# Spreading the four store transfers of a transposed group over four attention units, and one unit's sum moved ahead of another's shift

## The chip, the cores and the metric

The kernel runs on one core of one Trainium2 chip, alone. The metric is the device time of one execution in microseconds (us); the kernel before takes 838.05 us, the median of three runs (835.47, 838.05 and 839.6). The profile is of one further execution, which took 836.59 us; 834.8 us of that is the span from its first to its last instruction.

## The reference, cut to what matters

Three stages follow each other. Attention: 4 batches, 8 heads, 768 positions, head size 64, in chunks of 32 queries that see a window of 64 keys (8 memory keys, 16 on the left, the chunk itself, 8 on the right).

```python
scores = scale * np.matmul(q_c, k_full.transpose(0, 1, 3, 2))
scores = scores - np.max(scores, axis=-1, keepdims=True)
a = np.exp(scores)
a = a / (np.sum(a, axis=-1, keepdims=True) + 1e-09)
out[:, :, c_start:c_end] = np.matmul(a, v_full)
```

Its output, as x with 3072 tokens of 512 features, goes through two dense blocks:

```python
h = x @ w_in                                   # 512 -> 1024
solu = h * softmax(h)
ln = (solu - mean) / np.sqrt(var + 1e-06) * g_ln
x = ln @ w_out                                 # 1024 -> 512
g = np.maximum(0.01 * (x @ w_in2), x @ w_in2)  # 512 -> 2048
out = g @ w_out2                               # 2048 -> 512
```

## The kernel before, in words

The attention is cut into 32 units of work: eight blocks of 384 tokens times four pairs of heads. The first dense product (step `hidden`), the softmax and the normalization run over 24 tiles of 128 tokens, three per block. Every fp32 product of the dense blocks is made of three products of split operands (high and low parts).

All engines take their work from one list of steps, written out by hand: `START` for the first block, `BLOCK_STEPS` for each further block, `TAIL` for the end (lines 106 to 202). `schedule()` puts them together, and each engine walks the same list and does the steps that it has in its own table (`run`, line 443). So the order within an engine is fixed, and engines meet only at semaphores.

One attention unit a goes like this. SyncE (SP) issues `load_q(a)`, `load_k(a)`, `load_v(a)`: 192, 384 and 384 KB. `load_q` goes to one of two buffers `q_raw`; the other two go to one of four slots of `attn_buf`. GpSimd (POOL) copies q into the slot with zeros between heads (`place_q`, line 1386, two copies at line 1399). TensorE (PE) makes the scores (line 695); VectorE (DVE) takes the maximum away (`shift`, lines 1139 to 1146); ScalarE (ACT) does `expo` (line 861); DVE sums and inverts (`rsum`, lines 1155 to 1157); POOL multiplies (`probs`, line 1407); PE transposes (`probs_t`, line 707); ACT spreads the result over a diagonal layout (`spread`); PE multiplies by the values (`values`, line 721); ACT and DVE take the high and low part of the result (`x_hi`, `x_lo`).

In `BLOCK_STEPS` POOL's work stands in this order for block t, counted in units from 4t: place 8, probs 4, place 9, probs 5, probs 6, place 10, place 11, probs 7, with the small steps of the normalization (`stats`, `stats_a`) between. POOL is in order, so a `place_q` that waits for its q holds up the `probs` behind it. SP is in order too: `load_v(a)` waits until `values(a-4)` has read the slot, `load_q(a)` until `place_q(a-2)` has read the buffer, `load_k(a)` until `scores(a-4)` is done.

After normalization DVE transposes each tile in squares of 32 (`tr`, line 1181) into `lnT`, which has two buffers of four tiles (a group, 2 MB). Six groups are written to DRAM: `store_ln(g)` (line 477) waits for the group's last transpose and issues four transfers, each of 32 partitions, 512 KB, with 512 bytes of contiguous DRAM per piece. `tr` of the first tile of group g+2 waits until all four transfers of group g have landed. In `schedule()` the whole `store_ln(g)` is put behind the first `scores` step that is more than 24 steps after the group's last `tr`; the last two groups are put directly behind their last `tr` in `TAIL`. `load_ln` later reads the groups back for the second dense product.

At the very beginning PE multiplies zeros (`keep_warm`, line 838) while the first loads arrive: 10, 6 and 12 matmuls, which the profile counts as 20, 12 and 24.

Of the kernel before, what the change touches and what calls it, by code (L numbers as in the profile page):

```python
# [22 lines left out]
P = 128  # L23
# [11 lines left out]
HALVES = TOKENS // HALF  # L35
NT = BLOCKS * TILES
GROUP = HALF // P
SQUARE = 32
# [63 lines left out]
def down_count(b, p, j=PAIRS2 - 1):  # L102
# [2 lines left out]

START = (
        ("keep_warm", 10), ("place_q", 0),
        ("scores", 0), ("keep_warm", 6), ("load_q", 4), ("load_k", 4), ("place_q", 1), ("shift", 0),
        ("scores", 1), ("keep_warm", 12), ("load_q", 5), ("load_k", 5), ("expo", 0), ("place_q", 2), ("shift", 1), ("rsum", 0), ("expo", 1), ("rsum", 1), ("probs", 0), ("w1_hi", 0), ("probs", 1),
        ("probs_t", 0), ("spread", 0), ("w1_lo", 0),  # L110
        ("scores", 2), ("load_q", 6), ("load_k", 6), ("place_q", 3),
        ("values", 0), ("load_v", 4), ("shift", 2),
# [94 lines left out]
def schedule():  # L207


    s = []  # L210

    def add(*steps):
        s.extend(steps)


    def x2_steps(h, k):
        add(("x2", h, k))
        if k == 3 and h >= 1:
            for m in range(KM):
                add(("stage_x2", h - 1, m))  # L220
            add(("store_x2", h - 1))
        if k % 2 == 1 and h + 2 < HALVES:
            add(("load_ln", h + 2, k // 2))
        if (h, k) == (2, 5):
            add(("load_w2", 0), ("load_w2", 1), ("load_t", 0, 0), ("load_t", 0, 1))
        elif h == 3 and k < 2:
            add(("t_sums", 0, k), ("store_t", 0, k))
        elif h == 3 and k in (3, 4):
            add(("w2_sum", k - 3))
        elif h == 3 and k in (5, 6):  # L230
            add(("w2_hi", k - 5), ("w2_lo", k - 5))
        elif (h, k) == (3, 7):
            add(("load_op", 0, 0), ("load_op", 0, 1), ("load_op", 0, 2))
        elif h == 4 and k >= 1:
            add(("operand", 0, k - 1))
            if k + 2 < OPERANDS:
                add(("load_op", 0, k + 2))
        elif (h, k) == (5, 0):
            add(("load_w2", 2), ("load_w2", 3))
        elif h == 5 and k in (3, 6):  # L240
            add(("w2_sum", 2 if k == 3 else 3))
        elif (h, k) == (5, 4):
            add(("w2_hi", 2), ("w2_lo", 2))

    add(("load_q", 0), ("load_k", 0), ("load_q", 1), ("load_k", 1), ("load_consts",), ("load_v", 0), ("load_w1", 0),
        ("load_q", 2), ("load_k", 2), ("load_v", 1), ("load_w1", 1), ("load_q", 3), ("load_k", 3), ("load_v", 2),
        ("load_w1", 2), ("load_v", 3), ("load_w1", 3))
    add(*START)


    waiting = []

    def with_stores(step):
        add(step)
        if step[0] == "tr" and step[1] % GROUP == GROUP - 1:
            waiting.append((step[1] // GROUP, len(s)))
        if waiting and step[0] == "scores" and len(s) > waiting[0][1] + 24:
            add(("store_ln", waiting.pop()[0]))

    for t in range(1, BLOCKS - 1):  # L260
        for kind, offset, *rest in BLOCK_STEPS:
            if kind in OF_UNIT:
                if t * HEAD_PAIRS + offset < UNITS:
                    with_stores((kind, t * HEAD_PAIRS + offset))
            elif kind in ("w1_hi", "w1_lo"):
                if t + offset < W1_PIECES:
                    add((kind, t + offset))
                    if (kind, t + offset) == ("w1_lo", KM):
                        add(("load_w1", W1_PIECES - 1))
            else:  # L270
                with_stores((kind, t * TILES + offset, *rest))
    for c in range(4):
        add(("load_ln", 0, c))
    for step in TAIL:
        if step[0] == "x2":
            x2_steps(*step[1:])
        else:
            add(step)
        if step == ("tr", NT - GROUP - 1):
            add(("store_ln", HALVES - 2))  # L280
            for c in range(4):
                add(("load_ln", 1, c))
        elif step == ("tr", NT - 1):
            add(("store_ln", HALVES - 1))

    for h in range(2, HALVES):
        for k in range(K1):
            add(("ln_hi", h, k), ("ln_lo", h, k))
            x2_steps(h, k)
    for m in range(KM):  # L290
        add(("stage_x2", HALVES - 1, m))
    add(("store_x2", HALVES - 1))

    return s


def build(nc, q_in, k_in, v_in, w1_in, w2_in, g_in, ident_in, out):
# [7 lines left out]
    def at(name, offset, shape, dt=f32):  # L305
        return nc.alloc_sbuf_tensor_at(name, shape, dt, offset=base + int(offset))
# [13 lines left out]
    lnT = [at(f"lnT{i}", (80 + 16 * i) * KB, [P, D_FF1 // SQUARE, GROUP, SQUARE]) for i in range(2)]  # L320
# [44 lines left out]
    ln_dram = nc.dram_tensor("ln_scratch", [HALVES, SQUARE, D_FF1 // SQUARE, HALF], f32, kind="Internal").ap()  # L365
# [6 lines left out]
    with ctx:  # L372
# [3 lines left out]
        def sem(name):  # L376
            return ctx.enter_context(nc.semaphore(name))
# [19 lines left out]
        s_ln_out = [sem(f"s_ln_out{i}") for i in range(2)]  # L397
# [41 lines left out]

        block = ctx.enter_context(nc.Block())  # L440
        steps = schedule()

        def run(table):
# [7 lines left out]
        def _(sp):  # L451
# [22 lines left out]
                    sp.wait_ge(s_w_lo, i - RAW + 1)  # L474
                sp.dma_start(raw[i % RAW][:, :], src).then_inc(s_raw[i % RAW], 16)

            def store_ln(g):
                sp.wait_ge(s_tr, GROUP * (g + 1))
                for i in range(P // SQUARE):
                    sp.dma_start(ln_dram[g, :, :, i * P:(i + 1) * P],  # L480
                                 lnT[g % 2][i * SQUARE:(i + 1) * SQUARE].rearrange("r c t n -> r c (t n)"))\
                      .then_inc(s_ln_out[g % 2], 16)

            def load_ln(h, c):
                if h == 0:
# [104 lines left out]
            def store_out(b, which, f):  # L590
# [3 lines left out]
                if which == 21 and b == SPANS - 1 and f == 1:  # L594
# [4 lines left out]

            run(dict(load_q=load_q, load_k=load_k, load_v=load_v, load_consts=load_consts,  # L600
                     load_w1=lambda i: load_raw(i, w1_in[i]), store_ln=store_ln, load_ln=load_ln,
                     load_w2=load_w2, store_x2=store_x2, load_t=load_t, store_t=store_t, load_op=load_op))

# [886 lines left out]
```

## Time and profile before

| what | value |
|---|---|
| median of three runs | 838.05 us (835.47 to 839.6) |
| the profiled execution | 836.59 us |
| its span | 834.8 us |
| mean granted TensorE clock | 0.995 |
| PE busy | 811.8 us, 97% |
| DVE busy | 544.4 us, 65% |
| ACT busy | 452.9 us, 54% |
| POOL busy | 97.5 us, 12% |
| DMA | 156.64 MB, 188 GB/s over the span |

Busy time of PE is the time in which a matmul was in flight, and it is pipelined; what it leaves out of the span are true pauses of PE. The attention with the first dense product takes the first 217 us or so. The profile's page cuts the span into 40 slices of 20.9 us; PE's busy share is 9 tenths or more in most of them and dips in the first four and in single later ones, and the granted clock dips in one (the seventh, 125 to 146 us).

### The profile page before, as it was taken

The page shows a single profiled execution, that of the slowest core. Times are in us where ns is not written, and L with a number is a line of the kernel's source. Part 1 is how long each engine was busy: PE and PEld are TensorE (multiplying, and loading weights), DVE is VectorE, ACT ScalarE, POOL GpSimd, SP SyncE. Part 2 cuts the span into 40 slices and gives each one's busy share as a digit, 9 for nine tenths or more (in the row PEclk, how much of TensorE's full clock was granted, in tenths as well). Part 3 has the DMA queues.
Part 4 walks back from the last instruction along what each step waited for, and adds up shares of the span by engine and source line. Part 5 has one row for each costly group of instructions (what it writes and reads, how often), then busy time and mean ns, then how long its engine had stood idle before and what let it go on. Part 6 is the DMA issues. An engine that isn't in the chain of part 4 may idle for free.

```text
span 834.8 us, 13082 instructions
## 1 busy us (share of the span) xinstructions
PE 811.8 (97%) x4856; PEld 659.4 (79%) x4856; DVE 544.4 (65%) x898; ACT 452.9 (54%) x729; POOL 97.5 (12%) x220
## 2 busy tenths in 40 slices
PE   8899997989999999999999999999899999999998
PEld 7767776767888888888888888888677888888886
DVE  7779795877743266616734335555778699769875
ACT  3567675656744335535555446456644554555553
POOL 4454344352210000000000000000000000000000
PEclk9999998999999999999999999999999999999999
DMA  9685866664675896426685468444950850274001
GB/s 341 220 284 157 243 180 182 179 203 124 180 241 125 314 340 210 145 101 228 214 293 180 182 216 298 161 170 164 326 190 26 292 188 26 81 260 138 26 1 75
DMA packets 84495, 156.64 MB, mean 188 GB/s; under 512 B 6736, under 2 KB 35536, under 8 KB 84432
## 3 DMA queue, kind: packets, MB, share of 16 engines
q1 hardware_dynamic: 84432, 155.81, 56.1%
q8 instruction: 38, 0.62, 0.3%
q14 instruction: 25, 0.20, 0.1%
HBM read 99.16 MB, written 56.62 MB: 187 GB/s over the span
## 4 chain that ended last, share of the span: by engine, by line
PE 85%; DVE 4%; issue 4%; DMA 3%; POOL 1%; ACT 1%; SPq 0%; POOLq 0%; DVEq 0%
PE hid_a L729 21%; PE hid_b L729 19%; PE scores_a L729 13%; PE attn_ps L729 13%; PE scores_b L729 8%; PE probs_ps L729 7%; PE attn_ps L721 2%; DMA g_blk<-g_scratch 1%; PE probs_ps L707 1%; PE scores_a L695 1%; PE scores_b L695 1%; DMA g_scratch<-g_out 1%; DVE ring_lo L1124 1%; DVE g_blk L1260 1%; DMA attn_buf<-k_in 1%
## 5 line engine op out<-in xcount | busy, mean ns | idle before, releaser
L855 ACT ACTIVATE ring_hi<-g_blk 128x512 fp32r<-128x512 f32 x168 | 105.9, 632 | 112.0 <-PE hid_a L729 41.2
L1124 DVE TENSOR_TENSOR ring_lo<-g_blk,ring_hi 128x512 fp32r<-128x512 f32 x168 | 115.4, 690 | 36.3 <-ACT ring_hi L855 33.1
L992 ACT ACTIVATE g_out<-g_out 128x512 f32<-128x512 f32 x72 | 45.4, 630 | 91.5 <-DVE g_out L1239 60.2
L729 PE MATMUL hid_b<-ring_hi,w_hi 128*128 128x512 f32 x128 | 50.2, 392 | 3.0 <-DVE ring_lo L1124 3.0
L729 PE MATMUL hid_b<-ring_hi,w_lo 128*128 128x512 f32 x128 | 49.8, 389 | 0.0
L729 PE MATMUL hid_b<-ring_lo,w_hi 128*128 128x512 f32 x128 | 49.8, 389 | 0.0
L729 PE MATMUL hid_a<-w_in_hi,xT_hi 128*128 128x512 f32 x96 | 41.5, 432 | 3.1 <-DVE u L1170 2.3
L729 PE MATMUL hid_b<-w_in_hi,xT_hi 128*128 128x512 f32 x96 | 40.5, 422 | 0.4 <-DVE xT_lo L1124 0.2
L1399 POOL COPY attn_buf<-q_raw 64x384 f32<-64x384 f32 x64 | 33.8, 528 | 48.4 <-DMA q_raw<-q_in 38.0
L855 ACT ACTIVATE diag<-probs_ps 64x384 f32<-64x384 f32 x64 | 30.9, 483 | 14.8 <-PE probs_ps L707 14.0
L1124 DVE TENSOR_TENSOR x_op_P_lo<-op_raw,x_op_P_hi 128x1024 fp32r<-128x1024 f32 x21 | 25.7, 1224 | 20.3 <-ACT x_op_P_hi L855 20.2
L729 PE MATMUL attn_ps<-x_op_P_hi,w_hi 128*128 128x512 f32 x96 | 37.7, 393 | 0.7 <-ACT g_out L855 0.7
L729 PE MATMUL hid_a<-w_in_hi,xT_lo 128*128 128x512 f32 x96 | 38.2, 398 | 0.0
L729 PE MATMUL hid_a<-w_in_lo,xT_hi 128*128 128x512 f32 x96 | 38.0, 396 | 0.0
L1124 DVE TENSOR_TENSOR w_lo<-w_raw,w_hi 128x1792 fp32r<-128x1792 f32 x16 | 32.3, 2020 | 8.7 <-ACT w_hi L855 8.7
L729 PE MATMUL hid_b<-w_in_hi,xT_lo 128*128 128x512 f32 x96 | 37.7, 393 | 0.0
L729 PE MATMUL scores_a<-x_op_P_hi,w_hi 128*128 128x512 f32 x96 | 37.5, 390 | 0.0
L729 PE MATMUL hid_b<-w_in_lo,xT_hi 128*128 128x512 f32 x96 | 37.4, 390 | 0.0
L729 PE MATMUL attn_ps<-x_op_P_hi,w_lo 128*128 128x512 f32 x96 | 37.4, 389 | 0.0
L729 PE MATMUL attn_ps<-x_op_P_lo,w_hi 128*128 128x512 f32 x96 | 37.4, 389 | 0.0
L729 PE MATMUL scores_a<-x_op_P_lo,w_hi 128*128 128x512 f32 x96 | 37.4, 389 | 0.0
L729 PE MATMUL scores_a<-x_op_P_hi,w_lo 128*128 128x512 f32 x96 | 37.3, 389 | 0.0
(205 smaller groups left out, 2152.5 us busy)
## 6 DMA issues: line engine op xcount, KB each, us to landing
g_scratch<-g_out SPq DMA_DIRECT2D x96, 256.0 KB, 2.4
g_blk<-g_scratch SPq DMA_DIRECT2D x48, 512.0 KB, 6.9
attn_buf<-k_in SPq DMA_DIRECT2D x32, 384.0 KB, 4.8
attn_buf<-v_in SPq DMA_DIRECT2D x32, 384.0 KB, 4.9
ln_scratch<-lnT SPq DMA_DIRECT2D x24, 512.0 KB, 6.9
w_raw<-w_in SPq DMA_DIRECT2D x16, 512.0 KB, 3.9
q_raw<-q_in SPq DMA_DIRECT2D x32, 192.0 KB, 4.6
ln_even<-ln_scratch SPq DMA_DIRECT2D x12, 512.0 KB, 6.5
```

The costliest lines, as they stand in the source:

```text
L695: mm = pe.matmul(scores_ps[a % 2][64 * p:64 * p + 64, pr * WINDOW:(pr + 1) * WINDOW], buf[:, c * 64:c * 64 + 64], buf[:, SEG + c * WINDOW: ...
L707: mm = pe.transpose(probs_ps[:, i * P:(i + 1) * P], prob[a % 2][:, i * P:(i + 1) * P], ident[:, :])
L721: mm = pe.matmul(tokens[64 * hb:64 * hb + 64, i, p], buf[:, 2 * SEG + n * HEAD_DIM:2 * SEG + (n + 1) * HEAD_DIM], dg[:, n, :, :], start=Tr ...
L729: mm = pe.matmul(psum, weights[i], data[j], start=first and n == 0, stop=last and n == 2, skip_group_check=goes_on)
L855: return act.activation(dst, src, ACT.Copy)
L992: act.activation(x, x, ACT.Prelu, alpha=0.01).then_inc(s_g[q], 1)
L1124: return ve.tensor_tensor(dst, x, hi.bitcast(f32), ALU.subtract)
L1260: ve.tensor_tensor(g_blk[11][:, j, :], g_blk[12][:, j, :], g_blk[11][:, j, :], ALU.add).then_inc(s_t2, 1)
L1399: op = pool.tensor_copy(padded[:, :, hb, :], q_raw[a % 2][rows, :].rearrange("d (c q) -> d c q", q=CHUNK))
```

## The change

Two things are changed in the order of steps; no instruction that computes the result is added or taken away.

First, `store_ln(g)` becomes `store_ln(g, i)`, one transfer each. For the groups that are stored within the blocks, the first transfer goes where the whole store went (behind the first `scores` that is more than 24 steps after the last `tr`), and each of the others behind one of the following `scores`. What is still waiting at the end of the blocks is put there, ahead of `load_ln(0, ...)`. Groups 4 and 5 keep their four transfers together. The semaphore counts are the same.

Second, in `START`, `rsum(0)` stands ahead of `shift(1)` instead of behind it, `probs(0)` ahead of `place_q(2)`, `expo(0)` with them; and `keep_warm` is called with 2 and 10 instead of 6 and 12.

```diff
         ("keep_warm", 10), ("place_q", 0),
-        ("scores", 0), ("keep_warm", 6), ("load_q", 4), ("load_k", 4), ("place_q", 1), ("shift", 0),
-        ("scores", 1), ("keep_warm", 12), ("load_q", 5), ("load_k", 5), ("expo", 0), ("place_q", 2), ("shift", 1), ("rsum", 0), ("expo", 1), ("rsum", 1), ("probs", 0), ("w1_hi", 0), ("probs", 1),
+        ("scores", 0), ("keep_warm", 2), ("load_q", 4), ("load_k", 4), ("place_q", 1), ("shift", 0), ("expo", 0), ("rsum", 0),
+        ("scores", 1), ("keep_warm", 10), ("load_q", 5), ("load_k", 5), ("shift", 1), ("expo", 1), ("probs", 0), ("place_q", 2), ("rsum", 1), ("w1_hi", 0), ("probs", 1),
...
-    waiting = []
+    waiting, after = [], [0]
 
     def with_stores(step):
         add(step)
         if step[0] == "tr" and step[1] % GROUP == GROUP - 1:
-            waiting.append((step[1] // GROUP, len(s)))
-        if waiting and step[0] == "scores" and len(s) > waiting[0][1] + 24:
-            add(("store_ln", waiting.pop()[0]))
+            waiting.extend((step[1] // GROUP, i) for i in range(P // SQUARE))
+            after[0] = len(s) + 24
+        if waiting and step[0] == "scores" and len(s) > after[0]:
+            add(("store_ln", *waiting.pop(0)))
...
+    for g, i in waiting:
+        add(("store_ln", g, i))
     for c in range(4):
         add(("load_ln", 0, c))
...
-            def store_ln(g):
+            def store_ln(g, i):
                 sp.wait_ge(s_tr, GROUP * (g + 1))
-                for i in range(P // SQUARE):
-                    sp.dma_start(ln_dram[g, :, :, i * P:(i + 1) * P],
-                                 lnT[g % 2][i * SQUARE:(i + 1) * SQUARE].rearrange("r c t n -> r c (t n)"))\
-                      .then_inc(s_ln_out[g % 2], 16)
+                sp.dma_start(ln_dram[g, :, :, i * P:(i + 1) * P],
+                             lnT[g % 2][i * SQUARE:(i + 1) * SQUARE].rearrange("r c t n -> r c (t n)"))\
+                  .then_inc(s_ln_out[g % 2], 16)
```

In the list that results, the four transfers of group 0 stand ahead of `load_q` 18, 19, 20 and 21, those of group 1 ahead of 23 to 26, those of group 2 ahead of 28 to 31. Of group 3 two stand among the last units and two at the end of the blocks; no other SP step stands between these four, nor between them and the `load_v(31)` ahead of them. The first transfer of every group stands where the whole store stood.

## Rows read from the trace of the kernel before

**Rows 1.** Who waited for whom, PE: us in total, times, longest us

```profile
PE probs_ps L707 <- POOL prob L1407: 8.1, 4, 4.3
```

**Rows 2.** Timeline of PE, the transposes of units 17, 18, 19, 21: start, us

```profile
117.05 0.55 PE L707 MATMUL probs_ps<-ident,prob 128*128 128x128 f32 x3
...
123.57 0.55 PE L707 MATMUL probs_ps<-ident,prob 128*128 128x128 f32 x3
...
134.49 0.90 PE L707 MATMUL probs_ps<-ident,prob 128*128 128x128 f32 x3 [4.32 <-POOL prob L1407]
...
149.95 0.55 PE L707 MATMUL probs_ps<-ident,prob 128*128 128x128 f32 x3
```

**Rows 3.** Timeline of PE, the transposes of units 23 and 24

```profile
163.01 0.55 PE L707 MATMUL probs_ps<-ident,prob 128*128 128x128 f32 x3
...
172.31 0.55 PE L707 MATMUL probs_ps<-ident,prob 128*128 128x128 f32 x3 [2.71 <-POOL prob L1407]
```

**Rows 4.** Busy time by stretch: engines, then PEclk, DMA share, GB/s

```profile
134.00:135.00 1.00, 0.52 (x3) 0.52 (x4) 0.00 (x0) 0.00 (x0) 0.81 (x3) 0.50 1.04 413
...
104.50:117.50 13.00, 13.00 (x140) 10.08 (x139) 12.18 (x23) 9.85 (x18) 6.54 (x14) 1.00 0.52 153
117.53:132.00 14.47, 12.64 (x136) 9.64 (x134) 12.89 (x27) 9.92 (x18) 2.80 (x8) 1.00 0.91 224
```

**Rows 5.** Timeline of POOL: the copies of q for units 18, 23, 28

```profile
98.33 1.04 POOL L1399 COPY attn_buf<-q_raw 64x384 f32<-64x384 f32 x2 [5.92 <-DMA q_raw<-q_in]
...
132.02 1.51 POOL L1399 COPY attn_buf<-q_raw 64x384 f32<-64x384 f32 x2 [9.91 <-DMA q_raw<-q_in]
...
170.31 1.04 POOL L1399 COPY attn_buf<-q_raw 64x384 f32<-64x384 f32 x2 [8.49 <-DMA q_raw<-q_in]
```

**Rows 6.** SP's queue: store 1's first transfer, load_q(23), each with its landing

```profile
117.53 0.56 SPq L480 DMA_DIRECT2D ln_scratch<-lnT  x1
DMA to landing us min/median/max: 5.0/5.0/5.0
...
123.57 2.51 SPq L455 DMA_DIRECT2D q_raw<-q_in  x1
DMA to landing us min/median/max: 8.4/8.4/8.4
```

**Rows 7.** Timeline of DVE: the first transpose of group 2

```profile
116.95 1.22 DVE L1181 STREAM_TRANSPOSE lnT<-u 128x1024 f32<-128x1024 f32 x1
```

**Rows 8.** Timeline of all engines at the start

```profile
1.03 4.63 PE L843 MATMUL hid_b<-lnT 128*128 128x128 f32 x20 [1.03 <-DVE lnT L1126]
...
8.45 0.52 ACT L861 ACTIVATE prob<-shifted 128x384 f32<-128x384 f32 x1 [6.45 <-DVE shifted L1146]
...
9.38 2.94 PE L843 MATMUL hid_b<-lnT 128*128 128x128 f32 x24
...
9.54 0.07 DVE L1139 MEMSET scores_b<- 64x16 f32 x1 [1.12 <-PE scores_b L695]
...
10.18 1.05 POOL L1399 COPY attn_buf<-q_raw 64x384 f32<-64x384 f32 x2 [2.93 <-issue]
...
10.71 0.54 DVE L1155 TENSOR_REDUCE unit_sum<-prob 128x6 f32<-128x384 f32 x1
...
10.82 0.52 ACT L861 ACTIVATE prob<-shifted 128x384 f32<-128x384 f32 x1 [1.86 <-DVE shifted L1146]
11.26 1.04 ACT L855 ACTIVATE w_in_hi<-raw 128x1024 fp32r<-128x1024 f32 x1
...
11.83 0.83 POOL L1407 TENSOR_TENSOR prob<-prob,unit_sum 128x384 f32<-128x384 f32 x1 [0.60 <-DVE unit_sum L1157]
...
12.80 0.52 PE L707 MATMUL probs_ps<-ident,prob 128*128 128x128 f32 x3 [0.47 <-POOL prob L1407]
...
13.36 0.99 ACT L855 ACTIVATE diag<-probs_ps 64x384 f32<-64x384 f32 x2 [1.06 <-PE probs_ps L707]
...
16.68 0.47 PE L729 MATMUL hid_a<-w_in_hi,xT_hi 128*128 128x512 f32 x1 [0.79 <-DVE xT_lo L1124]
```

More of the change, by code:

```diff
@@ L279, in schedule @@
         if step == ("tr", NT - GROUP - 1):
-            add(("store_ln", HALVES - 2))
+            for i in range(P // SQUARE):
+                add(("store_ln", HALVES - 2, i))
             for c in range(4):
@@ L283, in schedule @@
         elif step == ("tr", NT - 1):
-            add(("store_ln", HALVES - 1))
+            for i in range(P // SQUARE):
+                add(("store_ln", HALVES - 1, i))
     for h in range(2, HALVES):
```

## The prediction

> **What bounds the kernel now.** I read the page first: PE is busy for 97% of the span and the chain that ended last is 85% PE, so what can be won without taking matmuls away is only what PE loses in pauses. Next I asked who PE waited for. One line stands out: the transposes of `probs_t` waited 8.1 us in four waits for POOL's `probs` [rows 1]; no other line has more than 3.0 us. Two of the four are in the body. In the timeline of PE the transposes come at a fixed beat, 123.57 - 117.05 = 6.52 us a unit, with nothing idle between [rows 2], until that of unit 19 waits 4.32 us; that of unit 24 waits 2.71 us [rows 3].
>
> The reader should follow such a wait back. POOL's `probs` of unit 19 stands behind `place_q(23)`, which began at 132.02 after 9.91 us of waiting for its q; that of unit 24 stands behind `place_q(28)`, which waited 8.49 us [rows 5]. In SP's queue `load_q(23)` was to go at about 117.5, but the store of group 1 stood ahead: the first of its four transfers was issued at 117.53, `load_q(23)` at 123.57, and it then took 8.4 us to land [rows 6]. So q was late twice over: 6.0 us in SP's queue, where the later stores issue slowly because the DMA queues are full, and then behind 2 MB in the DMA engines. Group 2's store does the same to q 28. Group 0's store holds q 18 back as well (5.92 us of waiting until 98.33) [rows 5], but there a slower part of POOL's list follows and PE is not reached.
>
> **The stores, part by part.** What the two pauses cost is more than their length. After the long one the granted clock is 0.50, the 1.2 GHz level [rows 4]. I take the cost from the beat: from the transpose of unit 18 to that of unit 21 are three beats, 19.56 us; it took 149.95 - 123.57 = 26.38, so 6.82 us were lost, 4.32 in the wait and 2.50 at half clock. For unit 24: 172.31 - 163.01 - 6.52 = 2.78 us, no clock lost. Together 9.60 us. PE has no further wait in the rest of the attention, so nothing gives these back later: the beat is PE's own.
>
> What do the spread transfers need? Each unit then has, in SP's order: `load_v` (which waits for `values`), one transfer of the store, `load_q`, and `load_k` behind its scores. The first transfer took 0.56 us to issue when nothing was queued ahead and 5.0 us to land [rows 6]. So `load_q(23)` goes at about 118.1 instead of 123.57, 5.4 us sooner, and its q lands behind one transfer, at 118.1 + 6 = 124. Even with the 8.4 us of before it would be there at 126.5. Its deadline: the transpose of unit 19 is due at 130.09, less 0.83 for `probs` and 1.05 for the two copies, that is 128.2. That leaves 4 us, 1.7 us at the worst. For q 28 there is more, since its deadline is the seventh beat behind 123.57 (169.2) less 1.9, and its load goes at about 157.5. For the second to fourth transfer of a group the pattern repeats a beat later each; the four loads that they stand ahead of had no such delay before, and each now gets 0.6 us in SP's queue and one transfer's time in the DMA engines. The tightest of them is q 19, which has the place in POOL's list of q 23 and so the same 4 us. So I take all 9.60 us.
>
> Can the engines carry it? Without a store a unit's loads keep the DMA engines busy for 0.52 of the time, 3.4 us of 6.52 [rows 4]. A transfer costs between 2.3 us (0.524 MB at the 224 GB/s of the crowded stretch) [rows 4] and 3.1 us (the first landed at 122.5 and q 23 at 132.0 [rows 6], with three transfers and q between: 9.4 / 3). A unit with a transfer takes 5.7 to 6.5 us of 6.52. It fits at both ends, at the upper one with nothing to spare, and every fifth or sixth unit has no transfer.
>
> DVE must not be made to wait: `tr(8)` needs all of group 0 landed. The fourth transfer now goes three beats after 84.9, at about 104.5 to 105, and lands by 111 to 114 even at the slowest landing of a store (9 us would be 114); `tr(8)` starts at 116.95 [rows 7]. For groups 1 and 2 the next user is four and more beats after the fourth transfer's issue. Group 3's transfers have no other SP step between them, and groups 4 and 5 are untouched, so the tail is as before. The 18 more steps on SP each repeat a wait that is long satisfied: nothing.
>
> **The start.** `expo(0)` starts at 8.45, takes 0.52, so DVE can sum at 9.0 while it now idles until 9.54 [rows 8]. `rsum(0)` takes about 1.0 us (10.71 until POOL starts at 11.83, with the hand-over). `shift(1)` then starts at 10.0 instead of 9.54, and `expo(1)` at 11.26 instead of 10.82. POOL does `probs(0)` at 10.1 to 10.9 instead of 11.83, and `place_q(2)` behind it, until 12.0. The shorter `keep_warm` calls (2 and 10) let PE arrive at the transpose at about 11 instead of 12.3; it runs at 11.1 instead of 12.80, 1.7 us sooner. But that isn't what comes last. `spread(0)` on ACT stands behind `expo(1)` and `w1_hi(0)`, which takes 1.04; it starts at 11.26 + 0.45 + 1.04 = 12.75, against 13.36. From there values, `x_hi`, `x_lo` and the first `hidden` follow as before, so the 16.68 becomes 16.1. The gain is 0.6 us; its bounds are 0 (a later load, whose issue time hangs on nothing that moves, eats it) and 1.7 us (the whole of the transpose's advance). I take 0.6, since ACT's order sets it.
>
> The sum is 9.6 + 0.6 = 10.2 us. Against the profiled execution: 836.6 - 10.2 = 826.4. The median of the runs is 1.5 us above that execution, which gives 827.9. Part of the 4 us by which the three runs differ may be the pauses themselves, which would go with them; I take the middle, 827.1.
>
> **The rivals.** (A) One pause stays in part. Deciding point: q lands over 4 us later than I have it. Then the smaller, 2.78 us, stays or the long one turns into one of that kind: 829.9 to 831. For it: the upper price of a transfer leaves no slack. Against it: even the 8.4 us landing fits.
>
> (B) The stores aren't the cause, and q is late for lack of its buffer. Then only the start moves: 837.5. Against it: the issue times in [rows 6] show 6 us spent on store transfers right ahead of the load.
>
> (C) Slower: single transfers occupy the engines for longer than four in a row. In the rows a lone transfer needs 5.0 us to land, and consecutive ones are at most 3.1 us apart. Should the engines be taken for the whole 5.0, a unit would need 3.4 + 5.0 = 8.4 us against 6.52; after four units q would be 7.5 us late, 3.5 past its slack, with 2.5 us at half clock in each of three groups: 18 us in the place of 9.6, so 836.6 - 10.2 + 18 = 844. It decides from 3.1 us a transfer upwards. Against it: a landing time is mostly latency, during which the engines serve the next transfer. The Trainium skill (DMA: Bandwidth & Descriptors, Rules for kernel authors) speaks for this rival: it asks for at least 1 MiB in a DMA for full bandwidth; by it, lone transfers of 512 KB would use the engines badly. No row here shows that for stores this far apart.
>
> (D) The clock comes late at the start. The first 20 warm-up records took 4.63 us, 0.23 each, the last 24 took 2.94, 0.12 each [rows 8], which is half and full rate. With 12 of the 56 records gone and PE idle for about 0.5 and 1 us behind the transpose, the array might fall back; the hidden products up to 20 us would then cost up to 3.5 us more: 830.6. Against it: the pause of 2.71 us at unit 24 left the clock alone. The Trainium skill (TensorE: Matmul & The Clock Gate, Part 1) says that the full clock has to be earned by sustained work and that the moment varies from run to run, which speaks against taking warm-up matmuls away; [rows 4] agree only in that a long idle time costs the clock.
>
> **How the numbers follow.** Chances: forecast 0.70, A 0.12, D 0.06, B 0.07, C 0.05. Range: from 824.2 (the fastest run, 835.5, less 9.6, less the upper 1.7 of the start is 824.2) to 831.5 (A and D); outside are B and C and little else. About 0.5%, 4.2 us, is what a measurement of this kernel can tell from no change. The forecast, A and D are beyond it on the fast side: together 0.88; B is within: 0.07; C beyond on the slow side: 0.05.
>
> **What would show it.** The transposes of units 19 and 24 on the beat, with PE's wait for `probs` in the body gone and no slice with a lower clock; load_q 23 issued near 118 and landed by 125; single `ln_scratch` transfers a beat apart, each issued in well under 1 us; the first `hidden` at about 16.1 with `probs_t(0)` at about 11.1. Wrong would be: POOL waiting for q longer than 5 us just ahead of a `probs`, DVE waiting at `tr(8)`, or a rise of the DMA share to 1.0 over several beats.

## The result, and the profile after

The changed kernel takes 826.25 us, the median of six runs (824.33 to 827.06), against 836.76 us for the kernel before beside it (834.9 to 839.6, six runs). The ratio is 0.9863 with a 95% interval of 0.9846 to 0.9879: 10 to 13 us faster. I had forecast 827.1 us, between 824.2 and 831.5. Two executions of the changed kernel in a later set took 1002.26 us (at a mean granted clock of 0.753) and 2059.39 us; all medians and ratios here leave them out.

The profiled execution took 824.33 us with a span of 822.5 us; it is the fastest of the six. The granted clock is 1.000 where it was 0.995, DMA moves the same 156.64 MB. Who waited for whom, PE, in the changed kernel (us in total, times, longest):

```profile
PE hid_b L733 <- DVE ring_lo L1128: 2.9, 4, 1.2
PE hid_a L733 <- DVE u L1174: 2.6, 2, 1.6
PE probs_ps L711 <- POOL prob L1411: 1.1, 2, 0.8
PE hid_b L847 <- DVE lnT L1130: 1.0, 1, 1.0
PE scores_b L699 <- POOL attn_buf L1403: 1.0, 1, 1.0
```

The wait for `probs` has gone from 8.1 us to 1.1 [rows 1], and what is left of it lies in the first 40 us. The transposes of units 17 to 20 in PE's timeline answer to [rows 2]; they now keep the beat of 6.52 us throughout:

```profile
115.33 0.55 PE L711 MATMUL probs_ps<-ident,prob 128*128 128x128 f32 x3
...
121.86 0.55 PE L711 MATMUL probs_ps<-ident,prob 128*128 128x128 f32 x3
...
128.38 0.55 PE L711 MATMUL probs_ps<-ident,prob 128*128 128x128 f32 x3
...
134.91 0.55 PE L711 MATMUL probs_ps<-ident,prob 128*128 128x128 f32 x3
```

SP's queue at the same place, with the landing of each (compare [rows 6]): the first transfer of group 1, `load_q(23)` right behind it, then the second transfer, a beat later, and `load_q(24)`:

```profile
115.81 0.57 SPq L484 DMA_DIRECT2D ln_scratch<-lnT  x1
DMA to landing us min/median/max: 5.1/5.1/5.1
...
116.42 2.86 SPq L460 DMA_DIRECT2D q_raw<-q_in  x1
DMA to landing us min/median/max: 5.0/5.0/5.0
...
122.34 0.56 SPq L484 DMA_DIRECT2D ln_scratch<-lnT  x1
...
122.94 0.66 SPq L460 DMA_DIRECT2D q_raw<-q_in  x1
DMA to landing us min/median/max: 6.0/6.0/6.0
```

q 23 is there 5.6 us behind the place of the store; before, it took 14.4 us. By stretch (length; busy PE, PEld, DVE, ACT, POOL; clock, DMA share, GB/s), a unit without and one with a transfer:

```profile
108.91:115.44 6.53, 6.53 (x70) 5.07 (x71) 5.01 (x11) 4.30 (x8) 2.25 (x6) 1.00 0.49 151
121.97:128.49 6.52, 6.52 (x70) 5.06 (x71) 5.48 (x12) 5.58 (x11) 2.73 (x8) 1.00 0.80 227
```

The difference in the DMA share, 0.31 of 6.52 us, is 2.0 us for one transfer of 512 KB.

At the start the profiled execution is ahead of the forecast: the first hidden product begins at 14.72, not 16.1. The timeline of PE shows why:

```profile
1.03 3.88 PE L847 MATMUL hid_b<-lnT 128*128 128x128 f32 x20 [1.03 <-DVE lnT L1130]
...
4.85 0.92 PE L699 MATMUL scores_a<-attn_buf 128*64 128x64 f32 x24
...
14.72 0.47 PE L733 MATMUL hid_a<-w_in_hi,xT_hi 128*128 128x512 f32 x1 [0.58 <-DVE xT_lo L1128]
```

The same 20 warm-up records took 4.63 us in the kernel before [rows 8], and the first scores 1.47 us instead of 0.92: the matmuls came to their full rate sooner here. This is read from their durations alone, since the granted clock reads 1.00 from the start in both traces. It is no work of the change, since nothing ahead of it differs.

### The profile page after: what moved, and what is told of

The parts are those of the page before. It is cut to its first block, busy times and chain, and to the rows that moved or that the text cites. A ratio compares the mean times of both kernels' runs of the same rounds, so it can differ in the third digit from the quotient of the medians.

```text
span 822.5 us, 13059 instructions
## 1 busy us (share of the span) xinstructions
PE 806.6 (98%) x4844; PEld 654.9 (80%) x4844; DVE 545.1 (66%) x898; ACT 453.2 (55%) x729; POOL 97.1 (12%) x220
## 2 busy tenths in 40 slices
DMA packets 84495, 156.64 MB, mean 190 GB/s; under 512 B 6736, under 2 KB 35536, under 8 KB 84432
## 4 chain that ended last, share of the span: by engine, by line
PE 90%; DVE 3%; DMA 2%; issue 1%; POOL 0%; ACT 0%; SPq 0%; DVEq 0%; POOLq 0%
PE hid_a L733 22%; PE hid_b L733 21%; PE scores_a L733 13%; PE attn_ps L733 13%; PE scores_b L733 8%; PE probs_ps L733 7%; PE attn_ps L725 3%; PE probs_ps L711 2%; PE scores_a L699 1%; DMA g_blk<-g_scratch 1%; PE scores_b L699 1%; DMA g_scratch<-g_out 1%; DVE g_blk L1264 1%; DVE ring_lo L1128 1%; DVE neg_max L1170 0%
## 5 line engine op out<-in xcount | busy, mean ns | idle before, releaser
L893 ACT ACTIVATE e<-u,neg_mean 128x1024 f32<-128x1024 f32 x24 | 27.5, 1147 | 13.5 <-DVE neg_mean L1177 13.4
```

Source lines behind the costliest of these rows:

```text
L893: act.activation(e1[n % 2][:, :], u[n % 3][:, :], ACT.Square, bias=neg_mean[:, n:n + 1], accum_out=sq_sum[:, n:n + 1]).then_inc(s_square, 1)
```

## The experiments

My theory: the two pauses of PE are made by the store standing ahead of `load_q(23)` and `load_q(28)`, and a pause begins only where q lands later than 10.7 us behind the store's place (the prediction's deadline of 128.2 less 117.5, where the store stood). The rivals: the gain comes from the start; any burst of 2 MB costs; a transfer is so dear for the DMA engines that the spread works only just.

**The two halves alone.** The START list of before in the changed kernel, and the other way round.

```diff
-        ("scores", 0), ("keep_warm", 2), ...
+        ("scores", 0), ("keep_warm", 6), ...   # the two lines of START as before; store_ln spread
```

> The changed kernel with the START list of before: only the stores are spread. Theory (the two pauses of PE come from q queued behind the store's 2 MB): both pauses gone, 9.6 us less than before, ratio 0.9885; the transposes of units 19 and 24 on the beat of 6.52 us, the first hidden product at 16.1 to 16.7 us as in the kernel before. Rival (the gain came mostly from the start, or from the clock rising earlier in the profiled execution): less than 6 us, ratio above 0.993.

> The kernel before with the START list of the changed one: stores four at a time. Theory: both pauses stay (waits of PE for probs of about 4.3 and 2.7 us at units 19 and 24), the gain is the start's 0.6 us at equal clock and up to 2 us where the clock happens to rise earlier: ratio 0.9975 to 0.9995. Rival (gain mostly from the start): over 4 us, ratio under 0.995.

The stores alone: 826.59 us against 837.29, ratio 0.9872 (0.9853 to 0.9892), PE with no wait at all between 60 and 230 us. The start alone: 837.46 us, ratio 1.0002 (0.9986 to 1.0018); the 0.9975 to 0.9995 that I had expected for it lies largely within this interval, so the run neither shows the 0.6 us nor rules them out. So the stores give all that can be measured, 10.7 us. The timeline of PE in the kernel with the start alone still has both pauses, and in this execution the second costs clock too:

```profile
123.78 0.55 PE L707 MATMUL probs_ps<-ident,prob 128*128 128x128 f32 x3
134.43 0.55 PE L707 MATMUL probs_ps<-ident,prob 128*128 128x128 f32 x3 [4.05 <-POOL prob L1407]
142.43 0.55 PE L707 MATMUL probs_ps<-ident,prob 128*128 128x128 f32 x3
148.96 0.55 PE L707 MATMUL probs_ps<-ident,prob 128*128 128x128 f32 x3
...
162.01 0.55 PE L707 MATMUL probs_ps<-ident,prob 128*128 128x128 f32 x3
171.75 0.55 PE L707 MATMUL probs_ps<-ident,prob 128*128 128x128 f32 x3 [3.15 <-POOL prob L1407]
179.74 0.55 PE L707 MATMUL probs_ps<-ident,prob 128*128 128x128 f32 x3
```

By the beat of 6.52 us: 148.96 - 123.78 - 19.56 = 5.6 us and 179.74 - 162.01 - 13.04 = 4.7 us, 10.3 together, where the profiled execution of before gave 9.6. The runs with the pauses lie 5.4 us apart (834.7 to 840.1 with the start alone), those without 0.9 us (826.22 to 827.13 in four for the stores alone) and 2.7 us (824.33 to 827.06 in six for the changed kernel). That the pauses vary, and so widen the spread, is likely but not shown by so few runs.

The changed kernel itself beside a third set of runs:

> The changed kernel itself, beside the next three on one chip. Theory (the stores give all of it, the start nothing that lasts, as the two halves done alone suggest): ratio 0.985 to 0.989, within 1 us of the stores alone (826.6). Rival (the halves help each other): 824.5 or less, ratio under 0.985.

Its ratio is 0.9859 (0.9834 to 0.9884), 826.07 us, the median of four, no different from the stores alone. The halves don't help each other by anything that can be measured.

**How many transfers may stand ahead of one load_q.** Two and two, then three and one, instead of one in each of four units.

```diff
-            add(("store_ln", *waiting.pop(0)))
+            for _ in range(2):                  # and: 3 if len(waiting) == 4 else 1
+                add(("store_ln", *waiting.pop(0)))
```

> The changed kernel with two transfers of a group ahead of each of two load_q instead of one ahead of each of four. Theory (what counts is when q lands against a deadline 10.7 us behind the place of the first transfer, and two transfers take about 4 us of the DMA engines): load_q 23 is issued about 1.2 us behind the first transfer and lands 7 to 8 us behind it, 3 us ahead of the deadline; no pause, time as the changed kernel, ratio 0.985 to 0.989. Rival (one transfer a unit is what makes it work, any crowding of a unit over 6.52 us of engine time gives a pause): a unit with two transfers needs 3.3 + 4.0 = 7.3 us, q late, a pause of 1 to 3 us in each of three groups, ratio 0.990 to 0.996.

> The changed kernel with three transfers of a group ahead of the first load_q and the fourth ahead of the next. So far q landed 5.6 to 6.6 us behind the place of the store with one transfer ahead, 8 to 10.5 with two, 14.4 with four; the deadline for units 23 and 28 is 10.7 us. Theory (PE pauses by what lands past the deadline): q at 11.5 to 12.5 us, pauses of 1 to 2 us in groups 1 and 2, none in group 0, no clock lost: 3 us more than the changed kernel, 828.5 to 831, ratio 0.988 to 0.992. Rival (any burst that fills the queues costs a like pause, two transfers are the most that goes free because SP isn't blocked): pauses of 3 us and more with the clock lost, ratio above 0.994.

Two and two: 827.09 us, ratio 0.9882 (0.9861 to 0.9903). Three and one: 828.16 us, ratio 0.9895 (0.9876 to 0.9914). Both ratios lie where the theory had them. SP's queue with two transfers, and with three; then POOL's copy of q 23 and PE's transpose of unit 19 with three:

```profile
117.71 2.16 SPq L485 DMA_DIRECT2D ln_scratch<-lnT  x2
119.91 1.94 SPq L461 DMA_DIRECT2D q_raw<-q_in  x1
DMA to landing us min/median/max: 7.0/7.0/7.0
```

```profile
118.22 4.50 SPq L485 DMA_DIRECT2D ln_scratch<-lnT  x3
122.76 2.07 SPq L461 DMA_DIRECT2D q_raw<-q_in  x1
...
129.30 1.04 POOL L1404 COPY attn_buf<-q_raw 64x384 f32<-64x384 f32 x2 [6.51 <-DMA q_raw<-q_in]
...
131.31 0.55 PE L712 MATMUL probs_ps<-ident,prob 128*128 128x128 f32 x3 [0.45 <-POOL prob L1412]
```

| transfers ahead of load_q 23 | q there, behind the store's place | PE's wait at unit 19 |
|---|---|---|
| 1 (changed kernel) | 5.6 us | none |
| 2 | 119.91 + 7.0 - 117.71 = 9.2 us | none |
| 3 | 129.30 - 118.22 = 11.1 us | 0.45 us |
| 4 (kernel before) | 14.4 us | 4.32 us |

With three ahead, PE's wait is the time by which q is later than 10.7 us. With four, q is 3.7 us past it and PE waits 4.32; the copies of that q also took 1.51 us there instead of 1.04 [rows 5], which makes up most of the rest. With three I had expected pauses of 1 to 2 us and found less. With two, q came later than the 7 to 8 us that I had expected: `load_q` itself took 1.94 us to issue behind the two transfers, against 0.43 for a `load_q` with no transfer ahead. And two ahead are free only at unit 19. In that kernel PE waits 0.39 us for `probs` at unit 20, and in the third group 1.1 us for DVE's `u`, which three and one shows too.

**The burst kept, but where its q isn't urgent.** The four transfers together, ahead of `load_q` 18, 26 and 30.

```diff
-        if waiting and step[0] == "scores" and len(s) > after[0]:
-            add(("store_ln", *waiting.pop(0)))
+        if waiting and step[0] == "scores" and len(s) > after[0] and step[1] in (14, 22, 26, 30):
+            while waiting:
+                add(("store_ln", *waiting.pop(0)))
```

> The changed kernel with the four transfers of a group kept together as in the kernel before, but placed ahead of load_q 18, 26 and 30 instead of 18, 23 and 28: each of these units is third of its block, whose place_q has no probs right behind it in POOL's list. Theory (it isn't the burst that costs but whose q it delays; group 0's burst cost PE nothing in the kernel before): no pause over 1 us, time as the changed kernel, 826 to 828, ratio 0.984 to 0.989. Rival (a burst of 2 MB delays some probs wherever it stands): pauses of 2 to 4 us in two groups, ratio above 0.993.

827.34 us, ratio 0.9880 (0.9857 to 0.9903). The burst of group 1 blocks SP for 6 us and POOL waits 6.22 us for its q, as the timelines of SP and POOL show, and the only wait of PE for `probs` between 60 and 230 us is one of 0.4 us:

```profile
137.12 5.97 SPq L485 DMA_DIRECT2D ln_scratch<-lnT  x4
143.14 2.86 SPq L461 DMA_DIRECT2D q_raw<-q_in  x1
...
150.84 1.04 POOL L1404 COPY attn_buf<-q_raw 64x384 f32<-64x384 f32 x2 [6.22 <-DMA q_raw<-q_in]
```

This is the clearest of the runs: nearly the whole gain without spreading anything. What cost time was which q stood behind the burst. No run changed the other half of the chain, POOL's order: by the same reading, `probs` moved ahead of the waiting `place_q` should hide the late q as well, but that wasn't tried.

**The burst behind the loads of its unit.** Four together, behind `load_k` instead of ahead of `load_q`.

```diff
-        if waiting and step[0] == "scores" and len(s) > after[0]:
-            add(("store_ln", *waiting.pop(0)))
+        if waiting and step[0] == "load_k" and len(s) > after[0]:
+            while waiting:
+                add(("store_ln", *waiting.pop(0)))
```

> The changed kernel with the four transfers of a group kept together again, but queued behind load_q and load_k of the unit instead of ahead of them. Theory (q's own place in the queue decides): q 18, 23 and 28 land within 3 to 4 us; the next q (19, 24, 29) is issued some 6 us late and lands within 1 us of its deadline on either side: pauses of at most 1 us each, ratio 0.985 to 0.990. Rival (2 MB in one burst stalls the engines wherever it stands): the next unit's q takes over the delay, PE pauses of 2 us and more at units 20 and 25, ratio above 0.992.

830.15 us, ratio 0.9924 (0.9899 to 0.9949): slower than I had it, and on the rival's side of its mark of 0.992, though none of the pauses is as long as the 2 us that it named. q 23, 18 and 28 are in time, and the delay passes to the next unit, as the rival said. PE waits 2.7 us for `probs` in three waits, the longest 1.70 us where I had at most 1, and 1.7 us for `u`, so that the third group alone loses some 3.8 us by the beat. SP, POOL and PE of that kernel, and the step of ACT that makes `u`:

```profile
119.59 5.76 SPq L485 DMA_DIRECT2D ln_scratch<-lnT  x4
...
127.85 1.74 SPq L461 DMA_DIRECT2D q_raw<-q_in  x1
...
134.36 1.04 POOL L1404 COPY attn_buf<-q_raw 64x384 f32<-64x384 f32 x2 [5.81 <-DMA q_raw<-q_in]
...
136.37 0.55 PE L712 MATMUL probs_ps<-ident,prob 128*128 128x128 f32 x3 [0.32 <-POOL prob L1412]
...
168.80 1.04 POOL L1404 COPY attn_buf<-q_raw 64x384 f32<-64x384 f32 x2 [9.45 <-DMA q_raw<-q_in]
...
170.80 0.55 PE L712 MATMUL probs_ps<-ident,prob 128*128 128x128 f32 x3 [1.70 <-POOL prob L1412]
...
171.93 1.24 ACT L899 ACTIVATE u<-u,shift,gain 128x1024 f32<-128x1024 f32 x1 [7.85 <-POOL shift L1424]
```

In the third group the second wait follows, 1.71 us for DVE's `u` at 176.90: the late q has also held back the small steps of the normalization on POOL, which stand behind the copy. That path wasn't in my deadline.

**What a full queue costs.** Each transfer of groups 0, 1 and 2 issued twice, the second time to spare memory. The counts that others wait for are raised to match (left out here); no wait of DVE for a store came of it.

```diff
+                if g < 3:
+                    sp.dma_start(spare[g, :, :, i * P:(i + 1) * P],
+                                 lnT[g % 2][i * SQUARE:(i + 1) * SQUARE].rearrange("r c t n -> r c (t n)"))\
+                      .then_inc(s_ln_out[g % 2], 16)
```

> The changed kernel with every transfer of groups 0, 1 and 2 issued twice, the second time to spare memory: 6 MB more, two transfers ahead of each of the 12 load_q. Theory (a transfer takes the engines 2.0 us, as the DMA share of the changed kernel says: 0.80 against 0.49 of 6.52 us): a unit needs 3.2 + 4.0 = 7.2 us of 6.52, the backlog grows by 0.7 us a unit to some 3 us, q lands 7 to 10 us behind the first transfer's place against 10.7: no pause or pauses under 1 us, ratio 0.985 to 0.990. Rival C of the prediction (a transfer takes 3.1 us or more): 3.2 + 6.2 = 9.4 us a unit, backlog 3 us a unit, q 5 us and more past its deadline at the fourth unit of each group: pauses of 2 to 5 us in each group, ratio 0.995 to 1.01.

834.49 us, ratio 0.9953 (0.9937 to 0.9969), 8 us more than the changed kernel. The size that I expected was wrong and the ratio lies in the rival's range; by the beat the three groups lose 4.0, 1.1 and 4.3 us. The DMA share of two stretches of 6.5 us is close to full, and the transfers of successive units are 8.2 and 7.5 us apart on SP, longer than the beat. By stretch (columns as above), then the timelines of SP and PE:

```profile
88.50:95.00 6.50, 6.50 (x71) 5.04 (x70) 6.03 (x13) 4.21 (x8) 1.22 (x3) 1.00 0.98 264
101.50:108.00 6.50, 6.50 (x71) 5.04 (x70) 6.33 (x12) 5.53 (x9) 3.24 (x8) 1.00 0.97 244
```

```profile
91.43 0.56 SPq L486 DMA_DIRECT2D ln_scratch<-lnT  x1
...
99.67 0.56 SPq L486 DMA_DIRECT2D ln_scratch<-lnT  x1
...
101.00 3.82 SPq L462 DMA_DIRECT2D q_raw<-q_in  x1
...
107.14 0.56 SPq L486 DMA_DIRECT2D ln_scratch<-lnT  x1
...
111.91 0.55 PE L717 MATMUL probs_ps<-ident,prob 128*128 128x128 f32 x3 [1.33 <-POOL prob L1417]
...
176.63 0.55 PE L717 MATMUL probs_ps<-ident,prob 128*128 128x128 f32 x3 [2.21 <-POOL prob L1417]
```

With 7.85 us for a unit, the mean of the two, and 3.2 for its loads, a transfer takes about 2.3 us when the engines are full, against 2.0 when they aren't. (The other two groups have distances of 7.1 to 9.1 us, so this is an estimate to some tenths.) The price was nearly right; what I had left out is that SP stands still meanwhile (3.82 us for one `load_q`), so that each unit's loads are themselves issued a beat's excess (1.3 us) later than those of the unit before. Above full use lateness adds up in SP's order and isn't spread. Rival C's mechanism is real; the changed kernel, at 0.79 to 0.83 in its units with a transfer, stays below its point.

**The start.** The changed kernel without the second and third `keep_warm`; and with two copies of q moved ahead.

```diff
-        ("scores", 0), ("keep_warm", 2), ...
-        ("scores", 1), ("keep_warm", 10), ...
+        ("scores", 0), ("keep_warm", 0), ...
+        ("scores", 1), ("keep_warm", 0), ...
```

> The changed kernel without the second and third keep_warm (2 and 10 matmuls to none). Theory: PE has 0.9 us of work between about 6 and 10.6 us; the clock, which has just risen, falls back, the scores and transposes to 15 us don't care, but some of the hidden products behind 15 us run at half clock: 1 to 3.5 us more than the changed kernel, 827 to 830. Rival (idle time of this length costs no clock, as at unit 24 of the kernel before with 2.71 us): as the changed kernel, 826.3.

```diff
-        ("values", 1), ("load_v", 5), ("w1_lo", 1), ("probs", 2),
+        ("values", 1), ("load_v", 5), ("w1_lo", 1), ("probs", 2), ("place_q", 4), ("place_q", 5),
...
-        ("hidden", 0, 2), ("w1_lo", 3), ("place_q", 4),
-        ("probs_t", 3), ("place_q", 5),
+        ("hidden", 0, 2), ("w1_lo", 3),
+        ("probs_t", 3),
```

> The changed kernel with place_q(4) and place_q(5) of the START list moved ahead, to behind probs(2), where POOL is idle for 5 us. Theory (what the start gains is eaten between 26 and 40 us, because load_q(6) and the loads behind it wait for place_q(4) while the DMA engines stand idle from 24 to 28 us): load_q(6) is issued at about 22 instead of 26.4 to 28, the wait of scores for k is gone, and 0.5 to 2 us are gained over the changed kernel: 824.5 to 826. Rival (the stretch is bound by DVE's normalization, which the loads don't touch): load_q(6) earlier, but the wait for u stays at 2 to 3 us and the time at 826 to 826.6.

Without the warm-up matmuls: 826.49 us, ratio 0.9866 (0.9841 to 0.9891), as the changed kernel. The theory was right on the clock and wrong on the time. After 2.3 us of idle time ahead of the transpose of 10.53 the granted clock goes on at 1.00 to 12 us and then falls, and the first hidden products take 0.63 us instead of 0.40. Two stretches of that kernel (columns as above), and a row of PE's timeline:

```profile
14.00:16.00 2.00, 1.58 (x17) 1.08 (x15) 1.20 (x3) 0.88 (x2) 1.11 (x3) 0.50 1.03 409
18.00:20.00 2.00, 2.00 (x37) 1.35 (x37) 1.36 (x2) 0.17 (x2) 1.68 (x1) 0.71 1.04 395
```

```profile
16.57 0.63 PE L733 MATMUL hid_a<-w_in_lo,xT_hi 128*128 128x512 f32 x1
```

The time doesn't show this loss. At unit 9, where the beat has set in, the transpose begins at 65.30, which is within what the kernels that kept their clock there show (63.1 to 65.5). With the copies ahead: 826.44 us, ratio 0.9859 (0.9835 to 0.9883), nothing gained. `load_q(6)` goes at 23.70 as intended, but the copies take 4.03 us for four records there, twice their usual time, and `probs(3)` behind them is late; PE waits 1.73 us at the scores of 33.38. The rival of this run had it right: PE's wait for `u` stays, 2.9 us against 2.6 in the changed kernel, and the time lies in its 826 to 826.6. A row each of the timelines of SP, POOL and PE:

```profile
23.70 0.33 SPq L460 DMA_DIRECT2D q_raw<-q_in  x1
```

```profile
21.83 4.03 POOL L1403 COPY attn_buf<-q_raw 64x384 f32<-64x384 f32 x4 [3.05 <-DMA q_raw<-q_in]
```

```profile
33.38 0.68 PE L699 MATMUL scores_a<-attn_buf 128*64 128x64 f32 x15 [1.73 <-issue]
```

So what bounds the first 60 us stays open: not PE's clock, and the loads alone don't free it; that it is DVE's normalization, as the rival said, fits the wait for `u` but wasn't tested. (The page of before has PE below 9 tenths in the first two of its slices, not in the first four.) No run beat the changed kernel.

## Why the prediction was right

**The stores, 9.6 us forecast, 10.7 us measured alone.** The reading of the wait back from PE over POOL to SP's queue held at each step: q 23 was issued at 116.42, 0.6 us behind the store's place, landed 5.6 us behind it (6.5 forecast), and the transposes are on the beat. Costing the pauses by the beat, clock included, and not by the waits alone (7.03 us) was what brought the size right. The 1 us between 9.6 and 10.7 needs no cause: the interval of that run is 9.0 to 12.3 us, and the pauses differ between executions, 10.3 us in the one with the start alone.

The profiles show the term by itself if the start, which varies, is left out. From the transpose of unit 9 to that of unit 31 the kernel before takes 152.06 us (64.83 to 216.89), the changed kernel 142.49 (63.12 to 205.61): 9.57 us less. The other kernels against this 142.49:

| kernel | unit 9 to unit 31, more than 142.49 us |
|---|---|
| stores alone; no later warm-up; copies ahead | 0.0 |
| four together where q has slack | 0.9 |
| two and two | 1.8 |
| three and one | 2.0 |
| four behind the loads | 5.0 |
| every transfer doubled | 9.4 |
| the kernel before | 9.6 |
| the start alone | 10.7 |

**The deadline.** 10.7 us behind the store's place was right for q 23, within 0.1 us by the kernel with three ahead. For q 28 the prediction counted wrongly: unit 24 is six beats behind unit 18, not seven (39.16 us in the changed kernel, 121.86 to 161.02). Its 169.2 is near the right time in the trace of before only because the seventh beat stands in for the 6.8 us lost at unit 19, and with the load at 157.5 and 6 us for its way it leaves 3.8 us, the same slack as for q 23 and not more. This did no harm, since q 28 behaved like q 23. The deadline was also too narrow in one respect: POOL's normalization steps behind the copy have one too. It showed as a wait for `u` in the burst behind the loads, in the doubled transfers and, with 1.1 us, in two and two and three and one.

**The price of a transfer, 2.3 to 3.1 us forecast, 2.0 measured (2.3 in full queues).** This term was set too high. The upper end came from landings, which hold the waiting of other loads in them. The difference of two DMA shares, a unit with and one without, is the better reading, and it needs a unit with one transfer, which the kernel before doesn't have. Its rows give only the price in full queues: 14.47 us at 224 GB/s are 3.24 MB, of which 1.14 MB are loads, some 3.9 us at the price of the undisturbed stretch; that leaves 2.3 us of DMA time for each of the four transfers [rows 4], the lower end of my range. The error made the engines' room look smaller than it was (5.7 to 6.5 us of 6.52, for a measured 5.2 to 5.4) and gave weight to rivals A and C; no term of the sum hung on it.

**The start, 0.6 us forecast, nothing measurable.** The working holds as far as the first hidden product. When the full rate comes differs from execution to execution, so like must stand beside like, by the length of the first scores: with 1.47 us (before) the product began at 16.68, with 1.55 us (two and two) at 16.03, for a forecast of 16.1. With 1.21 us (stores alone) it was 16.42, with 1.32 us (doubled transfers) 15.80. But the lead of 0.6 us can't be made out at unit 9: its transpose begins at 64.8 and 65.5 with the START list of before and at 63.1 to 65.5 with the new one. The measurement of the half alone, 1.0002 (0.9986 to 1.0018), allows 0.6 us and allows none. Of the 12.3 us by which the profiled span is shorter, 1.7 us lie ahead of unit 9, 9.6 us between units 9 and 31, and 1.0 us behind, where a wait for `ring_lo` behind 600 us is that much shorter. The first and the last aren't shown to come from the change, and the profiled execution is the fastest of its six. The forecast was met by the stores' term; whether the start's 0.6 us belongs in the sum can't be told.

**The rivals.** A: no pause was left. B is out by the two halves: the stores alone take both pauses away, the start alone leaves both. C stands as a mechanism and, by the sum, begins above 6.52 - 3.2 = 3.3 us of transfers a unit, which is an estimate; with twice the transfers it costs 8 us. D: the profiled execution of the changed kernel keeps its clock (1.00 in every stretch of 5 us), and where the clock does fall, in the kernel without the later warm-up matmuls, no time is lost that can be measured (ratio 0.9866 beside 0.9859). The Trainium skill (TensorE: Matmul & The Clock Gate, Why this matters for your kernels) warns of idle gaps between bursts of matmuls; the trace agrees that the clock falls, to 0.50 between 13 and 19 us in the kernel without the warm-up matmuls, but there the time didn't follow.

## What to carry to other kernels

Where PE waits, follow the wait to the queue that is in order, and ask what stood ahead of the late load: here a store of 2 MB that nobody was waiting for yet. Compute the deadline of each load from the beat, and put bulk transfers where the load behind them has slack; a better place for all four, or two places instead of four, does nearly as well as an even spread (0.9 and 1.8 us more in the attention, of 9.6). Check that each beat's transfers stay below full use of the DMA engines, because above it the issuing queue fell behind by the excess, 1.3 us, at every beat.

## What was not expected of the hardware

A pause of 3.15 us cost clock in one execution (granted clock 0.50 from 174 to 176 us, and the next beat took 7.99 us instead of 6.52) and one of 2.71 us in another did not [rows 3]; in the start, 2.28 us of idle time after little work was enough. And two pairs of copies of q on POOL took 4.03 us, 2.0 us a pair, where a pair takes 1.04 us elsewhere; what slowed them wasn't tried.
